# Preparing a recurrence's decay tables on two engines instead of one, and issuing a dense layer's first products in another order

## The reference

```python
for t in range(S):
    kt, vt, rt = (k[:, :, t], v[:, :, t], r[:, :, t])
    cur = np.einsum('bhd,bhe->bhde', u[None] * kt, vt)
    y[:, :, t] = np.einsum('bhd,bhde->bhe', rt, state + cur)
    state = w[None, :, :, None] * state + np.einsum('bhd,bhe->bhde', kt, vt)
```

## Time and profile before

| what | value |
|---|---|
| median of 3 runs | 714.20 us (714.18 to 714.47) |
| the profiled execution: its time | 714.02 us |
| its span, first to last instruction | 712.2 us |
| PE busy | 697.3 us, 98% of the span |
| DVE, ACT, POOL busy | 387.2, 320.3, 139.4 us |
| mean granted TensorE clock | 1.000 |

### The profile page before, as it was taken

How to read it: one execution, slowest core, us unless ns; L and a number is a source line. 1 busy time by engine, 2 the same in 40 slices (tenths; PEclk the granted TensorE clock), 3 DMA queues, 4 the chain that set the end, 5 groups by cost and what they waited for, 6 DMA issues and landing times.

```text
span 712.2 us, 13909 instructions
## 1 busy us (share of the span) xinstructions
PE 697.3 (98%) x5202; PEld 634.1 (89%) x5202; DVE 387.2 (54%) x803; ACT 320.3 (45%) x699; POOL 139.4 (20%) x190
## 2 busy tenths in 40 slices
PE   7999999989999999999999999999999999999998
PEld 4888888879999999889999999999999999998997
DVE  6677677777878888675444333333333343334332
ACT  4776667725555555654433333333333333333222
POOL 9738666541322222100000000000000000000000
PEclk9999999999999999999999999999999999999999
DMA  9588776716666666410011002000200020001001
GB/s 189 129 201 188 168 171 145 228 48 241 224 217 239 207 232 228 135 42 1 0 42 49 0 1 89 1 0 1 90 0 1 1 90 0 1 1 45 1 1 44
DMA packets 106762, 65.71 MB, mean 92 GB/s; under 512 B 79764, under 2 KB 102296, under 8 KB 106704
## 3 DMA queue, kind: packets, MB, share of 16 engines
q1 hardware_dynamic: 102896, 60.31, 29.5%
q0 software_dynamic: 2560, 4.60, 2.0%
q10 hardware_dynamic: 1248, 0.02, 0.1%
HBM read 53.37 MB, written 12.48 MB: 92 GB/s over the span
## 4 chain that ended last, share of the span: by engine, by line
PE 92%; ACT 2%; DVE 2%; issue 1%; DMA 1%; another core or an unknown queue 1%; DVEq 0%; POOL 0%; SPq 0%; ACTq 0%; POOLq 0%
PE bank_A L964 8%; PE bank_A L965 8%; PE bank_A L963 8%; PE bank_L L963 4%; PE bank_L L965 4%; PE bank_L L964 4%; PE bank_P L964 4%; PE bank_P L965 4%; PE bank_P L963 4%; PE bank_A L880 4%; PE bank_kT L964 4%; PE bank_kT L965 4%; PE bank_kT L963 3%; PE bank_YT L965 3%; PE bank_YT L964 3%; PE bank_YT L963 3%
## 5 line engine op out<-in xcount | busy, mean ns | idle before, releaser
L1438 DVE TENSOR_TENSOR g_lo<-g,g_hi 128x512 fp32r<-128x512 f32 x96 | 66.5, 692 | 67.0 <-ACT g_hi L756 67.0
L756 ACT ACTIVATE g_hi<-g 128x512 fp32r<-128x512 f32 x96 | 60.7, 632 | 73.1 <-DVE g L1436 73.1
L1436 DVE SCALAR_TENSOR_TENSOR g<-cut,bank_A 128x512 f32<-128x512 f32 x60 | 41.3, 688 | 92.8 <-ACT cut L753 92.8
L753 ACT ACTIVATE cut<-bank_A 128x512 f32<-128x512 f32 x60 | 35.9, 598 | 101.3 <-PE bank_A L965 100.8
L965 PE MATMUL bank_A<-mT_hi,wi_lo 128*128 128x512 f32 x180 | 71.0, 394 | 0.0
L964 PE MATMUL bank_A<-mT_lo,wi_hi 128*128 128x512 f32 x180 | 70.9, 394 | 0.0
L627 ACT ACTIVATE bank_A<-ident,own 128x128 f32<-128x128 f32 x188 | 58.2, 357 | 27.5 <-DVE A_sb L1166 26.3
L963 PE MATMUL bank_A<-mT_hi,wi_hi 128*128 128x512 f32 x180 | 70.0, 389 | 0.0
L1436 DVE SCALAR_TENSOR_TENSOR g<-cut,bank_kT 128x512 f32<-128x512 f32 x36 | 24.8, 688 | 66.6 <-ACT cut L753 66.6
L753 ACT ACTIVATE cut<-bank_kT 128x512 f32<-128x512 f32 x36 | 21.5, 598 | 70.1 <-PE bank_kT L965 70.1
L963 PE MATMUL bank_kT<-mT_hi,wi_hi 128*128 128x512 f32 x108 | 42.1, 389 | 0.9 <-DVE mT_lo L1429 0.9
(11 more groups left out here) (271 smaller groups left out, 1854.5 us busy)
## 6 DMA issues: line engine op xcount, KB each, us to landing
raw<-in_moe_w_dram SPq DMA_DIRECT2D x24, 512.0 KB
raw<-in_moe_w_dram SPq DMA_DIRECT2D x7, 1536.0 KB
r_in<-in_r_dram SPq DMA_DIRECT2D x24, 192.0 KB, 3.7
k_in<-in_k_dram SPq DMA_DIRECT2D x24, 192.0 KB, 3.9
v_in<-in_v_dram SPq DMA_DIRECT2D x24, 192.0 KB, 3.3
x_scratch<-y_sb SPq DMA_DIRECT2D x24, 192.0 KB, 2.1
m_in<-x_scratch SPq DMA_DIRECT2D x5, 768.0 KB, 5.0
out_dram<-o_sb SPq DMA_DIRECT2D x10, 384.0 KB, 2.7
```

What stands on the lines that cost most here:

```text
L753: eng.activation(cut[f % 2][:, :], p_H[f % 3][:, :], ACT.Relu, bias=0.5, scale=1.0 / 6.0).then_inc(s_cut, 1)
L756: eng.activation(g_hi[f % 4][:, :], g[f % 2][:, :], ACT.Copy).then_inc(s_ghi, 1)
L1436: eng.scalar_tensor_tensor(g[f % 2][:, :], cut[f % 2][:, :], 1.0, p_H[f % 3][:, :], ALU.min, ALU.mult).then_inc(s_g, 1)
L1438: eng.tensor_tensor(g_lo[f % 4][:, :], g[f % 2][:, :], g_hi[f % 4][:, :].bitcast(F32), ALU.subtract).then_inc(s_glo, 1)
```

## The change

In the preparation of the recurrence:

- The two copies of `pw` (into the lower half of `powT_k`, and into `powT_r`) go from DVE to ACT. They raise a semaphore of their own, s_rev.
- The reciprocal is taken in two instructions of two head pairs each. PE transposes each half of `powT_k` by itself, the second into the bank L instead of kT; ACT copies each half out into its half of `w_k`; DVE multiplies each half of the first k by it. s_tabT, s_wk and s_k0 now count to 2. On ACT the copy into `powT_r` stands between the two halves of `w_k`; on DVE the reversed reciprocals (`powT_r`) stand between the two halves of `k_dec[0]`.
- k of batch 0 is issued from ACT's queue, right behind u; the four loads of the gate's weights go from ACT's queue to the end of SP's first loads.

In the dense pair: of the first piece of the first block the six matmuls that need only `mT_hi` are issued first, each kc behind s_mhi, and then the three that need `mT_lo`, each behind s_mlo. The number of matmuls is the same.

```diff
@@ -63,9 +63,11 @@
 N_PAR = 4
 N_CST = 7 + 3 * B
 TAB_U = 2
-TAB_K = TAB_U + NPAIR + 2
-TAB_R = TAB_K + 2
+TAB_PW = TAB_U + NPAIR
+TAB_K = TAB_PW + 2
+TAB_R = TAB_K + 1
 TAB_DONE = TAB_R + 2
+PART = NPAIR // 2
 
 
 def routed(group, steps):
@@ -116,6 +118,7 @@
         p_first = piece_of_L(B * E).rearrange("p (b e) -> p b e", b=B)
         p_logit2 = p_kT[:, 0:2 * B * E].rearrange("p (b e) -> p b e", b=B)
         p_countA = p_P[:, 2 * B * E:2 * B * E + (B + 1) * E].rearrange("p (b e) -> p b e", b=B + 1)
+        p_decays = [p_kT[:, 0:PART * P], p_L[:, 0:PART * P]]
         p_own = p_A[:, 0, 0:2 * TH].rearrange("p (t x) -> p t x", t=TH)
         p_countB = p_A[:, 1, 0:(B + 1) * E].rearrange("p (b e) -> p b e", b=B + 1)
         by_head = p_X.rearrange("p (h e) -> p h e", h=H)[:, :, 0:HD]
...
@@ -345,11 +349,17 @@
             wv = w.rearrange("(q two) d -> two d q", two=2)
             for o in range(2):
                 eng.dma_start(decay[HALF * o:HALF * o + HD, :], wv[o], allow_slow_non_contiguous=True).then_inc(s_w, 16)
-            load_rk(0, 0)
+            eng.dma_start(r_in[0][:, :, 0:HD], rows(r, 0, 0)).then_inc(s_rkin[0], 16)
             for b in range(1, B):
                 load_rk(b, 0)
                 load_v(b - 1, 0)
             load_v(B - 1, 0)
+            eng.wait_ge(s_cst, 4)
+            gate_by = w_gate.rearrange("(q o e) x -> o e q x", q=NPAIR, o=2)
+            skip_by = w_skip.rearrange("(q o e a) -> o e q a", q=NPAIR, o=2, a=1)
+            for o in range(2):
+                eng.dma_start(gate_w[HALF * o:HALF * o + HD, :, 0:E], gate_by[o]).then_inc(s_par, 16)
+                eng.dma_start(gate_w[HALF * o:HALF * o + HD, :, E:E + 1], skip_by[o], allow_slow_non_contiguous=True).then_inc(s_par, 16)
             eng.wait_ge(s_tok, 2)
             eng.dma_start(slots_by_p, nowhere[:, :, :]).then_inc(s_empty, 16)
             wo_dram = w_out.rearrange("(g p) n -> p g n", p=P)
@@ -361,7 +371,7 @@
                         eng.wait_ge(s_rtr, n + 1)
                         eng.wait_ge(s_rk, n + 1)
                         if n == 0:
-                            eng.wait_ge(s_k0, 1)
+                            eng.wait_ge(s_k0, 2)
                         load_rk(b, c + 1)
                     if n > 1:
                         b0, c0 = (n - 2) % B, (n - 2) // B
@@ -481,7 +491,7 @@
                 eng.wait_ge(s_rkin[b], 32 * (c + 1))
                 if not first:
                     if isinstance(c, int) and c == 0:
-                        eng.wait_ge(s_wk, 1)
+                        eng.wait_ge(s_wk, 2)
                     wait(eng, s_P, n - 3)
                     eng.tensor_tensor(k_dec[b][:, :, 0:HD], k3, w_k[:, :, 0:HD], ALU.mult).then_inc(s_kdec, 1)
                 wait(eng, s_ruk, n)
@@ -601,17 +611,19 @@
             uv = u.rearrange("(q two) d -> two d q", two=2)
             for o in range(2):
                 eng.dma_start(u_t[HALF * o:HALF * o + HD, :], uv[o], allow_slow_non_contiguous=True).then_inc(s_u, 16)
-            eng.wait_ge(s_cst, 4)
-            gate_by = w_gate.rearrange("(q o e) x -> o e q x", q=NPAIR, o=2)
-            skip_by = w_skip.rearrange("(q o e a) -> o e q a", q=NPAIR, o=2, a=1)
-            for o in range(2):
-                eng.dma_start(gate_w[HALF * o:HALF * o + HD, :, 0:E], gate_by[o]).then_inc(s_par, 16)
-                eng.dma_start(gate_w[HALF * o:HALF * o + HD, :, E:E + 1], skip_by[o], allow_slow_non_contiguous=True).then_inc(s_par, 16)
-
+            eng.dma_start(k_in[0][:, :].rearrange("s (h d) -> s h d", h=H), rows(k, 0, 0)).then_inc(s_rkin[0], 16)
+
+            eng.wait_ge(s_tab, TAB_PW)
+            eng.activation(powT_k[:, :, 0:HALF - 1], pw[:, :, HALF - 2::-1], ACT.Copy).then_inc(s_rev, 1)
             eng.wait_ge(s_uT, 1)
             eng.activation(u_all[:, :, :], by_head, ACT.Copy).then_inc(s_uall, 1)
-            eng.wait_ge(s_tabT, 1)
-            eng.activation(w_k[:, :, :], p_kT.rearrange("t (h d) -> t h d", h=H), ACT.Copy).then_inc(s_wk, 1)
+            for part in range(2):
+                own_h = slice(part * H // 2, (part + 1) * H // 2)
+                eng.wait_ge(s_tabT, part + 1)
+                eng.activation(w_k[:, own_h, :], p_decays[part].rearrange("t (h d) -> t h d", h=H // 2), ACT.Copy).then_inc(s_wk, 1)
+                if part == 0:
+                    eng.wait_ge(s_zero, 6)
+                    eng.activation(powT_r[:, :, HALF + 1:P], pw[:, :, 0:HALF - 1], ACT.Copy).then_inc(s_rev, 1)
 
             def k_transposed(b, c):
                 n, i = c * B + b, b % 2
@@ -801,10 +813,12 @@
                 last = eng.transpose(p_X[:, q * P:(q + 1) * P], u_less[:, q:q + 1].to_broadcast([P, P]), ident[:, :])
             last.then_inc(s_uT, 1)
             busy(2)
-            eng.wait_ge(s_tab, TAB_K)
-            for q in range(NPAIR):
-                last = eng.transpose(p_kT[:, q * P:(q + 1) * P], powT_k[:, q, :], ident[:, :])
-            last.then_inc(s_tabT, 1)
+            for part in range(2):
+                eng.wait_ge(s_tab, TAB_PW + part + 1)
+                eng.wait_ge(s_rev, 1)
+                for q in range(PART):
+                    last = eng.transpose(p_decays[part][:, q * P:(q + 1) * P], powT_k[:, part * PART + q, :], ident[:, :])
+                last.then_inc(s_tabT, 1)
             eng.wait_ge(s_cst, N_CST)
 
             def transposes(b, c):
@@ -1080,9 +1094,17 @@
                     eng.wait_ge(s_g, G2 * blk + (f - 1 if f < 2 else f - 2) + SHIFT)
                     if first:
                         eng.wait_ge(s_wilo, f + 1)
+                    if first and f == 0:
+                        for kc in range(KC):
+                            eng.wait_ge(s_mhi, kc + 1)
+                            eng.matmul(p_H[0][:, :], wi_hi[:, kc, 0:P], mT_hi[i][:, kc, :], start=kc == 0, stop=False)
+                            eng.matmul(p_H[0][:, :], wi_lo[:, kc, 0:P], mT_hi[i][:, kc, :], start=False, stop=False)
+                        for kc in range(KC):
+                            eng.wait_ge(s_mlo, kc + 1)
+                            a = eng.matmul(p_H[0][:, :], wi_hi[:, kc, 0:P], mT_lo[i][:, kc, :], start=False, stop=kc == KC - 1)
+                        a.then_inc(s_H, 1)
+                        continue
                     for kc in range(KC):
-                        if first and f == 0:
-                            eng.wait_ge(s_mlo, kc + 1)
                         piece = slice(f * P, (f + 1) * P)
                         a = three(p_H[f % 3][:, :], wi_hi[:, kc, piece], wi_lo[:, kc, piece],
                                   mT_hi[i][:, kc, :], mT_lo[i][:, kc, :], kc == 0, kc == KC - 1)
@@ -1132,18 +1154,28 @@
             assert done[0] == TAB_U
             for q in range(NPAIR):
                 tab(eng.tensor_tensor_scan(pw[:, q, :], decay[:, q:q + 1].to_broadcast([P, HALF]), ones[:, 0:HALF], 1.0,
-                                           ALU.mult, ALU.mult), free=q < NPAIR - 1)
-            tab(eng.reciprocal(powT_k[:, :, HALF:P], pw[:, :, :]), free=True)
-            tab(eng.tensor_copy(powT_k[:, :, 0:HALF - 1], pw[:, :, HALF - 2::-1]))
+                                           ALU.mult, ALU.mult), free=True)
+            assert done[0] == TAB_PW
+            for part in range(2):
+                own_q = slice(part * PART, (part + 1) * PART)
+                eng.wait_ge(s_tab, TAB_U + (part + 1) * PART)
+                tab(eng.reciprocal(powT_k[:, own_q, HALF:P], pw[:, own_q, :]), free=True)
             assert done[0] == TAB_K
-            tab(eng.tensor_copy(powT_r[:, :, HALF + 1:P], pw[:, :, 0:HALF - 1]), free=True)
+            eng.wait_ge(s_cst, N_CST)
+            eng.wait_ge(s_rkin[0], 32)
+
+            def first_decay(part):
+
+                own_h = slice(part * H // 2, (part + 1) * H // 2)
+                eng.wait_ge(s_wk, part + 1)
+                eng.tensor_tensor(k_dec[0][:, own_h, 0:HD], k_in[0][:, :].rearrange("s (h d) -> s h d", h=H)[:, own_h, :], w_k[:, own_h, 0:HD],
+                                  ALU.mult).then_inc(s_k0, 1)
+
+            first_decay(0)
+            eng.wait_ge(s_tab, TAB_K)
             tab(eng.tensor_copy(powT_r[:, :, 0:HALF], powT_k[:, :, P - 1:HALF - 1:-1]), free=True)
             assert done[0] == TAB_R
-            eng.wait_ge(s_cst, N_CST)
-            eng.wait_ge(s_wk, 1)
-            eng.wait_ge(s_rkin[0], 32)
-            eng.tensor_tensor(k_dec[0][:, :, 0:HD], k_in[0][:, :].rearrange("s (h d) -> s h d", h=H), w_k[:, :, 0:HD],
-                              ALU.mult).then_inc(s_k0, 1)
+            first_decay(1)
 
             def r_transposed(b, c):
                 n, i = c * B + b, b % 2
@@ -1305,6 +1337,7 @@
 
             current(0)
             eng.wait_ge(s_tab, TAB_R)
+            eng.wait_ge(s_rev, 2)
             r_transposed(0, 0)
             eng.wait_ge(s_seed, 1)
             eng.wait_ge(s_c, 1)
```

(3 more changed lines are left out.)

## The result

| | kernel before | with the change |
|---|---|---|
| median | 714.47 us (11 runs, 713.66 to 714.87) | 717.18 us (11 runs, 714.90 to 717.60) |
| profiled execution | 714.02 us | 717.19 us |
| its span | 712.2 us | 715.4 us |
| its mean granted clock | 1.000 | 0.995 |
| start of PE's products of step 1 | 16.77 us | 18.98 us |

The ratio of the two is 1.003, with a 95% interval of 1.0021 to 1.0040: slower, by 2.7 us, and outside the range that was given. The runs lie in groups. Three are at 714.90 to 714.98 us with a granted clock of 1.000, two at 716.55, six at 717.2 to 717.6, and these last eight have clocks of 0.993 to 0.995. The eleven runs of the kernel before lie within 1.2 us of each other, and its profiled execution has a clock of 1.000.

What follows compares the result with a forecast made beforehand. PE, busy in 98% of the span, was taken as the bound. Preparation −0.5, dense 0 and transfers 0 against the profiled 714.02 gave 713.5, or 713.7 us on the median's scale; range 712.8 to 715.4.

Steps and rivals of the forecast that it cites:

- The dense piece: First dense matmul: held by PE's sequencer, not mT_lo, so it starts at 301.65 us again; 0 gained.
- Reciprocal, reversed copy, halves through PE and ACT: Preparation: reciprocal halves end at 5.75 and 6.6 us, ACT's copy is covered, w_k whole about 7.9 instead of 8.49.
- The moved transfers: Loads of k and the gate's weights on other queues: nothing gained; at most some 0.1 us either way on w.
- The first product on DVE: Preparation: DVE waits only for POOL's ruk; k_dec[0] whole at 8.6 instead of 9.14 us, gain 0.5 to 0.6.
- rival 1: Preparation: POOL steps in between DVE's halves, second half ends at 10.4 us; slower, 715.4 us; chance 0.25.
- Rival 2: Preparation: POOL steps in only once, DVE's second half ends at 9.55 us, 0.4 late; 714.65 us; chance 0.12.

Runs made afterwards that it cites:

- e1: The kernel before with the reordered first dense piece alone: 710.74 us against 710.76, ratio 1.000.
- e8: The changed kernel with k of batch 0 on SP and the gate's loads on ACT as before: 710.23 us against the change's 710.27.
- e14: The changed kernel with POOL's product for step 1 waiting for both halves of k_dec of step 0, run again: 708.86 us, ratio 0.9985.
- e2: The changed kernel without the dense reordering: 710.34 us against the kernel before's 710.76, ratio 0.9995.
- e5: The changed kernel again without an edit, on the quick kind of chip: 710.27 us against the kernel before's 710.78, ratio 0.9997.
- e9: The changed kernel again without an edit, on the other kind of chip: 715.21 us against the kernel before's 714.72, ratio 1.001.
- e10: The changed kernel without the 3 nought matmuls ahead of the first k transposes: 717.09 us against the kernel before's 714.72, ratio 1.0027.
- e11: The changed kernel with 10 more nought matmuls ahead of step 0 and 16 more filler transposes at the tokens' wait: 715.93 us, ratio 1.0013.
- e4: The changed kernel with 13 instead of 3 nought matmuls ahead of the first k transposes: 710.44 us, ratio 0.9997.
- e13: The changed kernel once more without an edit: 711.36 us against the kernel before's 709.48, ratio 1.0008.
- e3: The changed kernel with POOL's product for step 1 waiting for both halves of k_dec of step 0: 710.08 us against 710.76, ratio 0.999.
- e6: The kernel before with 44 instead of 28 filler transposes at the wait for the first expert's tokens: 709.42 us against 710.78, ratio 0.998.

## Why the prediction was wrong

- *The dense piece: right.* Term 0, measured 0 (e1), and the semaphore is ruled out: the view of waits now names `mT_hi` in place of `mT_lo`, with the same 0.9 us, although `mT_hi` was ready 1.0 us before. That it is the sequencer's branches is read from its rows, in both kernels; no run takes the branches away.
- *Reciprocal, reversed copy, halves through PE and ACT: right to 0.1 us.* The first half of `w_k` is done at 7.19 (forecast 7.2), the second at 7.77 (7.9).
- *The moved transfers: put at nothing, right in the median only.* e8 shows no difference there. But k on ACT's queue lands 0.4 us earlier and so lets POOL start its `rk` and `ruk` ahead of DVE's first half, which put step 1 at 17.87 instead of 17.38 us in the profiled executions. This was not in the text.
- *The first product on DVE: wrong, and this is the step that failed.* The forecast had "the first half ends at about 8.3, the copy of the reciprocals takes 0.2 more, the second half 0.25". (These terms add up to 8.75, not to the 8.6 that the text took; e14, where the order was the forecast's, has 8.76.) The first half ended at 8.28; then POOL's product went first, as rival 1 had it, and the second half ended at 10.36 (rival: 10.4). The reason I gave against it, that DVE issues the next before the last has ended, is no reason: whoever waits goes next, in both directions. The row for it, `w_128` getting in ahead of a POOL product, was in the text and was given too little weight. So was the rule of the Trainium skill, page "SBUF — State Buffer", on who interferes with whom, that the engine that starts first holds the shared ports for its whole instruction; the trace agrees with it, in five instructions in a row.
- *Rival 1's price: right as far as it goes.* 715.4 was forecast for it. The three runs at clock 1.000 are at 714.9 to 715.0, though none of them was profiled; by e2 and e5 the turns cost 1.0 us at step 1 (17.87 against 16.77 to 16.87), and some 0.4 us of what comes later than before is won back by the tokens' arrival.
- *Rival 2: its order came too, and its price fits.* The order was that of e9 and e10, with the second half ending at 9.46 and 9.47 us (forecast 9.55). e9 is also the only measurement of the change on the other kind of chip beside the first, and its four runs at 1.000 are at 714.7 to 715.1 (forecast 714.65).
- *The clock: missing from the sum and from every rival.* Each case of mine that lengthened PE's idle time was priced at the upper clock. The fall costs 1.0 to 1.1 us ahead of step 0 (e10; 18.98 against 17.87) and 1.4 at the tokens. With these added to rival 1's 715.4 the range would have had to reach 717.9, and slower by over 0.2% would have deserved far more than the 0.08 that it got. That the share of runs with a fall differs from chip to chip could not be read from one execution.

The size of the first measurement's loss was partly chance. The same kernel came out at 1.001 (0.9998 to 1.0022) of the kernel before on the same kind of chip (e9) and within 0.1% of it on the quick kind; in the first measurement eight of eleven runs had clocks of 0.995 or less, which in the profiled executions goes with two falls.

What stays open: why the clock falls in some runs and not in others with the same idle time, where it fell in e11, what splits the runs at clock 1.000 into two groups, and what the change does on the other kind of chip once POOL waits.

## What to carry to other kernels

Where two engines exclude each other for a whole instruction, count turns and not durations. Splitting an instruction in two, or moving another between the halves, can give the other engine one more turn of its full length each time, unless it is made to wait for the last half. A transfer that lands earlier can cost time if it frees the competitor first. And when a change lengthens an idle time of the matmul engine, price what stands behind it at the lower clock too, and look whether the filler lasts until the wait ends.

## What the runs showed of the hardware that was not expected

- In the profiled executions PE's clock fell to 1.2 GHz behind idle times of 1.9 to 2.3 us (the first measurement, e4, e8, e10, e13) and did not fall behind others of 1.9 to 2.4 us (e1, e2, e3, e5, e9, e14). Once it fell where PE had idled only 0.5 us (e9).
- The kernel before's own runs lie in two groups on the quick kind of chip (709.1 to 709.5 and 710.6 to 712.1), 1 to 3 us apart, which is more than the change's effect there; 16 filler transposes at the tokens' wait took the group with the lower clock away (e6).
- In the changed kernel a start of 0.04 us earlier or later (7.04, 7.08) decided which engine went first, and so about 0.8 us (e9, e5).
